# Linear attention and two feed-forward blocks on one core: weight loads, output copies and a normalisation placed earlier in their queues

## The reference

```python
# attention with decay, per head: blocks of 64 tokens, a state carried from block to block
intra = einsum(einsum(qb, kb) * Dmask, vb);  inter = einsum(qb * lam_pow, kv_state)
out[block] = intra + inter
kv_state = lam_block * kv_state + einsum(kb * rev_pow, vb)
# first feed-forward block, on x of shape (2, 768, 512)
mixed = real(fft(fft(x, axis=1), axis=2))
u = x + mixed
un = (u - mean(u)) / sqrt(var(u) + 1e-6)
x1 = u + maximum(un @ w_ch1, 0) @ w_ch2          # 512 -> 2048 -> 512
# second feed-forward block
xn = (x1 - mean(x1)) / sqrt(var(x1) + 1e-6) * g_ln
y = x1 + maximum(xn @ w_ch1', 0) @ w_ch2'
```

## Time and profile before

| | |
|---|---|
| three runs, us | 577.79, 576.11, 578.07 |
| median | 577.79 |
| profiled execution, its own time | 577.79 |
| span of the profiled execution | 575.6 |
| PE busy | 565.5 us (98%) |
| PE weight loads | 390.2 us (68%) |
| DVE busy | 355.9 us (62%) |
| ACT busy | 245.6 us (43%) |
| POOL busy | 167.2 us (29%) |
| DMA engines | nearly full to 86 us; 59.85 MB moved in all |

### The profile page before, as it was taken

The page is one execution under the profiler, slowest core; times in us unless marked ns, Lnnn a source line. Parts: engine busy times, 40 slices in busy tenths (PEclk is TensorE's granted clock), DMA queues, the critical chain, the costliest instruction groups (busy, mean ns, idle before and its releaser), DMA issues.

```text
span 575.6 us, 10716 instructions
## 1 busy us (share of the span) xinstructions
PE 565.5 (98%) x4028; PEld 390.2 (68%) x4028; DVE 355.9 (62%) x618; ACT 245.6 (43%) x483; POOL 167.2 (29%) x147
## 2 busy tenths in 40 slices
PE   9899999999999999999999999999999999999997
PEld 5799987665666666666666666666666666666663
DVE  3446898998866776647969676975265533422223
ACT  1245676647763233424456454544232443232231
POOL 0668940775600011012295312620004300000000
PEclk9999999999999999999999999999999999999999
DMA  7999991000247437630235422132000223200001
GB/s 220 395 368 371 398 289 41 2 19 0 38 74 193 120 124 151 147 109 3 74 91 136 121 75 75 36 74 56 1 2 2 54 47 102 74 2 0 1 1 73
DMA packets 78515, 59.85 MB, mean 104 GB/s; under 512 B 39418, under 2 KB 65666, under 8 KB 77060
## 3 DMA queue, kind: packets, MB, share of 16 engines
q1 hardware_dynamic: 76260, 54.49, 33.2%
q10 hardware_dynamic: 1728, 3.15, 1.4%
q0 software_dynamic: 480, 1.57, 0.8%
HBM read 43.73 MB, written 6.30 MB: 87 GB/s over the span
## 4 chain that ended last, share of the span: by engine, by line
PE 79%; DVE 10%; issue 4%; DMA 3%; POOL 2%; ACT 1%; SPq 1%; DVEq 0%; ACTq 0%; POOLq 0%
PE bank L681 36%; PE bank L661 32%; PE bank L478 3%; PE bank L489 2%; PE bank L540 2%; DMA arena<-attn 2%; DVE arena L1341 2%; DVE arena L1179 2%; DVE arena L1181 2%; PE bank L448 2%; DVE arena L1188 1%; PE bank L461 1%; PE bank L605 1%; DVE arena L1306 1%; DVE arena L1386 1%
## 5 line engine op out<-in xcount | busy, mean ns | idle before, releaser
L681 PE MATMUL bank<-arena 128*128 128x512 f16 x1152 | 287.2, 379 | 1.4 <-DVE arena L1188 1.2
L661 PE MATMUL bank<-arena 128*128 128x256 f16 x2016 | 259.2, 273 | 1.0 <-DVE arena L1318 0.4
L661 PEld LDWEIGHTS bank<-arena 128*128 128x128 f16 x2016 | 196.4, 98 | 76.3 <-DVE arena L1386 1.8
L681 PEld LDWEIGHTS bank<-arena 128*128 128x128 f16 x1152 | 112.3, 98 | 88.2 <-DVE arena L1188 1.8
L1341 DVE SCALAR_TENSOR_TENSOR arena<-arena 128x512 f16<-128x512 f32 x96 | 74.1, 772 | 58.9 <-ACT arena L939 58.8
L939 ACT ACTIVATE arena<-arena 128x512 f16<-128x512 f32 x96 | 60.4, 629 | 104.7 <-DVE arena L1386 99.3
L1380 DVE SCALAR_TENSOR_TENSOR arena<-bank,arena 128x256 f32<-128x256 f32 x48 | 20.2, 421 | 62.3 <-PE bank L661 62.1
L1570 POOL TENSOR_TENSOR arena<-arena 128x512 f32<-128x512 f32 x12 | 18.6, 1570 | 88.8 <-DVE arena L1306 88.8
L1318 DVE TENSOR_TENSOR arena<-arena 128x512 f16<-128x512 f32 x42 | 34.3, 827 | 10.2 <-ACT arena L916 9.9
L991 ACT ACTIVATE arena<-bank 128x256 f32<-128x256 f32 x48 | 18.2, 380 | 48.6 <-PE bank L661 48.6
L1386 DVE SCALAR_TENSOR_TENSOR arena<-bank,arena 128x256 f32<-128x256 f32 x48 | 20.2, 420 | 25.9 <-PE bank L661 25.9
(11 more groups left out here) (112 smaller groups left out, 536.3 us busy)
## 6 DMA issues: line engine op xcount, KB each, us to landing
arena<-w SPq DMA_DIRECT2D x48, 256.0 KB, 4.2
arena<-w SPq DMA_DIRECT2D x24, 512.0 KB, 4.9
arena<-attn SPq DMA_DIRECT2D x10, 1024.0 KB, 8.4
out<-arena SPq DMA_DIRECT2D x12, 256.0 KB, 2.4
arena<-attn SPq DMA_DIRECT2D x4, 512.0 KB, 4.3
x_near<-arena ACTq DMA_DIRECT2D x6, 256.0 KB, 6.2
x_far<-arena ACTq DMA_DIRECT2D x6, 256.0 KB, 6.1
arena<-c SPq DMA_DIRECT2D x1, 1153.5 KB, 9.1
```

The lines of the kernel that those rows point to most:

```text
L661: last = nc.tensor.matmul(bank_, wst[:, i, wx, w, kt, :], xs[s % 2][:, x, ux, :, kt, :], start=not started and k == 0, stop=k == 5, skip_g ...
L681: last = nc.tensor.matmul(ops[t][:], hT[n % 2][:, half, hx, t * P:(t + 1) * P], wdn[:, i, wx, half * DM:(half + 1) * DM], start=first and ...
```

## The change

Four edits. (1) SP: each block c from 2 on gets two chunks of w1, chunk 2(c - 2) behind its queries and keys, chunk 2(c - 2) + 1 behind its values, so every chunk is issued one place earlier. (2) ACT: in units 0 to 5 `x_rows` stands ahead of `expand`. The table of magnitudes is replaced by one chunk per unit from unit 3, with chunks 6 and 7 at unit 9. (3) ACT, pair 4: the four `normal` tiles stand behind the copies of p1 and p7, instead of behind the two splits of the hidden rows. (4) ACT and DVE: block 0 of the next group is split in pair 4 behind the copy of p6, instead of in pair 5 behind that of p7.

```diff
-X_FIRST = {4: (1,), 5: (3,), 6: (5,)}, {5: (0, 1), 6: (3,), 7: (5,)}
-X_SECOND = {3: (0,), 4: (2,), 5: (4,), 6: (6,)}, {5: (2,), 6: (4,), 7: (6,)}
+X_FIRST = {4: (1,), 5: (3,), 6: (5,)}, {5: (1,), 6: (3,), 7: (5,)}
+X_SECOND = {3: (0,), 4: (2,), 5: (4,), 6: (6,)}, {4: (0,), 5: (2,), 6: (4,), 7: (6,)}
-MAGNITUDES = {3: (0,), 5: (1,), 6: (2,), 7: (3,), 8: (4, 5), 9: (6, 7)}
...
                 load_qk(c)
-                if c > 2:
-                    load_up(sp, 0, 2 * c - 5, wraw[0][:, 2 * c - 5, :], w_chunk_in[0][2 * c - 5])
+                load_up(sp, 0, 2 * (c - 2), wraw[0][:, 2 * (c - 2), :], w_chunk_in[0][2 * (c - 2)])
...
                 load_kv(c)
-                load_up(sp, 0, 2 * c - 4, wraw[0][:, 2 * c - 4, :], w_chunk_in[0][2 * c - 4])
+                load_up(sp, 0, 2 * (c - 2) + 1, wraw[0][:, 2 * (c - 2) + 1, :], w_chunk_in[0][2 * (c - 2) + 1])
                 if c == NBLK - 1:
-                    load_up(sp, 0, SLOTS - 1, wraw[0][:, SLOTS - 1, :], w_chunk_in[0][SLOTS - 1])
...
             for u in range(UNITS - 1):
-                if u < UNITS - B:
+                if u < B * HALF:
+                    x_rows(u)
                     expand(u)
-                x_rows(u)
-                for c in MAGNITUDES.get(u, ()):
-                    magnitude(0, c)
+                else:
+                    if u < UNITS - B:
+                        expand(u)
+                    x_rows(u)
+                if 3 <= u < 3 + SLOTS - 1:
+                    magnitude(0, u - 3)
+                if u == 2 + SLOTS - 1:
+                    magnitude(0, SLOTS - 1)
...
                 if n in LATE:
                     q_rows(LATE[n])
+                if n == 4:
+                    normal((0, 1))
                 act.wait_ge(p7_done, n + 1)
...
                     q_rows(4)
+                if n == 4:
+                    normal((2, 3))
...
                 hidden_hi(n, 1)
-                if n == 4:
-                    normal((0, 1))
...
                 hidden_hi(n, 0)
-                if n == 4:
-                    normal((2, 3))
```

## The result

| | before | after |
|---|---|---|
| median of 8 runs each, us | 577.84 | 581.63 |
| lowest to highest | 576.11 to 579.25 | 579.75 to 582.33 |
| ratio after / before | | 1.006 [1.0046, 1.0074] |
| profiled execution, its own time | 577.79 | 582.56 |
| its span | 575.6 | 580.8 |

The changed kernel is slower by 0.6%: +3.8 us by the medians, +3.5 by the ratio, whose interval reaches from 2.7 to 4.3. The forecast was +2.7 (580.5), slower. The time lies in the range. The terms behind it are another matter, and most of what follows is about them. The profiled execution, at 582.56, is slower than each of the eight.

The account below looks back on a forecast made before the run. TensorE (PE) sets the end, busy 98% of the span, so only its waits count. Terms 0.7 + 0.1 + 2.4 - 0.5 = +2.7 on 577.79 gave 580.5 us, range 577.6 to 582.9.

Parts of the forecast that it names:

- Term C: Normalised tiles in pair 4: ACT waits for shift, holding p7's eviction, so PE's p4 and p5 start late; +2.4 us.
- Term D: Feed-forward: POOL works in pair 4; PE waits 0.85 us in pair 5, not 1.33 in pair 6; -0.5 us.
- first rival: Pair 4's hold costs 2.4, pair 6's wait goes without successor, loads arrive in time: +1.1 us, 578.9, no change; chance 0.20.
- Term A: Attention: earlier w1 loads and x writes delay query/key and key/value blocks, so PE waits; +0.7 us, from 0 to 1.6.
- the deadlines: Attention: slack between landing and PE's first read of query/key blocks; landing 1.4 us later makes PE wait 0.55 for block 5.
- third rival: Attention loads not served in issue order, key/value block 1 delayed: +2.0 us, 581.8; chance 0.10 together with the high ends.
- Term B: First feed-forward group: POOL's last folds end later and meet DVE's first weight split; +0.1 us, from 0 to 0.5.
- second rival: Pair 4: DVE reaches shift 2.4 us earlier, all four waits of the first group go: -2.2 us, 575.6; chance 0.08.

Follow-up runs that it names:

- early shift: Pair 4's tile and block 0 moves, plus DVE's row_scale ahead of pair 3's w1 split, against the kernel before: 580.12 us against 579.91, ratio 1.0000.
- feed-forward run: Only pair 4's tile and block 0 moves, attention as before, against the kernel before: 580.33 us against 578.21, ratio 1.0019.

## Why the prediction was right, and where it was not

**What bounds the kernel.** Right: each change of PE's waits in the first group reached the end unchanged (3.0 us at pair 7, 3.0 at the last pair). The span grew by 5.2; the other 2.2 lie behind DVE's last instruction, where the last writes land (2.5 and 4.7 us). That part takes either of two lengths from one execution to the next, as said above, so one trace of each kernel can't put it down to the change.

**Term C (+2.4).** Right, mechanism and size. Tiles at shift's end, idle time put down to DVE, the p4 group 6.39 us after its pair's start where about 6.4 was forecast. The wait was 1.99 ahead of p4 and 0.20 ahead of p5; the pair grew by 2.56 with the clock at 1.0, in three traces (12.61 to 12.63). The early shift shows the cause. What the term lacked is the clock: in the first trace it fell to 0.50 after the wait and cost 1.3 more. No row of the trace of before could have given that, as the clock holds in its pairs.

**Term D (-0.5).** Sign right, size wrong: -1.40, just past the low end of its range, and the wait in pair 5 that it foresaw did not come. The step that failed is "POOL works at 141.7 to 148 instead, beside DVE's splits in pair 4". Only t1 moved. The chunk 7 sums behind it wait for DVE's split of chunk 5, which in pair 4 comes after the hold. In the second trace of the changed kernel, with the clock steady, PE wanted the w2 split at 149.70, where the forecast puts it (148.55, and 1.12 for the later start of pair 4), but the split ended at 149.20, and not at 150.5 (149.4, and 1.12). From the product eviction on, DVE took 5.2 us, not 6.6. In the kernel before, that split was done at 142.9 and POOL reached the sums only at 147.7, so its trace shows no wait there. But one chunk earlier it does, and the order could have been read from it (L1550 is the first sum of a chunk, L1181 the second half of DVE's w1 split):

```profile
134.07 1.05 POOL L1550 TENSOR_TENSOR arena<-arena 128x256 f32<-128x256 f32 x1 [0.94 <-DVE arena L1181]
```

The forecast took POOL's work as one block and left out what each of its instructions waits for. The first rival, which said that the wait of pair 6 goes without a successor, had this part right (and had given POOL's unchanged amount of work as the reason against it).

**DVE against POOL.** By the rule of the Trainium skill, "SBUF — State Buffer", section "Who interferes with whom", that a DVE instruction with two SBUF inputs and a GpSimd instruction that reads SBUF exclude each other, the prediction estimated about 2 us of wait in pair 5. No run shows one, as POOL did not work beside DVE's w1 split there. On the rule itself the prediction misread its row ("The row speaks for some overlap"). The lengths overlap, but the ends follow each other. POOL's sum of the earlier trace rows ends at 154.33 + 1.72 = 156.05, and DVE's split of the earlier trace rows at 157.13, 1.08 later: nearly the whole 1.28 that it takes alone still lay ahead of it. In the changed kernel POOL's L1553 ends at 148.23, DVE's L1191 at 149.31 (1.08 later), and POOL's L1554 at 149.89 (0.58 later; such a sum takes 0.72 alone). So the time for which an instruction is held lies inside its length.

All 14 traces say the same. In the first feed-forward group, a DVE instruction with both operands in SBUF (a split) began beside a running POOL instruction 138 times. In 112 of them it ended a fixed time after POOL did: 1.07 to 1.10 us for 1024 columns, 0.80 to 0.82 for 768, 0.53 to 0.56 for 512. In the other 26 DVE was done first, and POOL, though begun earlier, ended 0.58 to 0.60 after it. Here the two engines took turns, and the traces agree with the Trainium skill. DVE's evictions, which take one operand from PSUM, were not held: 104 of them that began beside POOL took 0.40 to 0.43, as L1383 at 142.66 beside L1586. The 6.9 us that the sum took from pair 5 of the kernel before held this taking of turns already, so the estimate of 2 us of wait counted part of it twice.

**Term A (+0.7).** Not seen, and not excluded. (The working itself comes to 0.6, since it says that the two delays don't add; 0.7 is a slip.) Edit 1 alone gives 0.9996, the rows' edit alone 0.9997, each with an interval of about 1 us to either side, and the Fourier part starts at the same mean time in traces with and without edit 1. The scores of block 5 stood at 52.86, and the prediction had named 52.8 as a sign of being wrong. The failing step is the deadlines: slacks of 1.5, 1.5 and 0.85 us were read from one execution. PE was to wait for block 5 and nowhere else; in the changed kernel it waited 0.31, 0.53 and 0.38 for blocks 3, 4 and 5. In others, with the order of loads of before, PE waits for blocks 4 and 5 too (0.46 and 0.67 in the feed-forward run). Landings vary by more than what the edit moves. Nor does the write of x, priced at 0.6 us ahead of key/value block 1, show: in the changed kernel PE's row group started at 20.83, 1.4 earlier than before, and over all traces its mean start is the same with and without the edit. For the third rival (+2.0 for the loads and writes) there is no sign either; edit 1's interval ends at +0.9.

**Term B (+0.1).** Pair 2 starts 49.8 us after the Fourier part in before and 50.3 in the changed kernel. Over all traces it is 50.4 with edit 1 (50.27 to 50.90) and 50.1 without (49.79 to 50.37), so about +0.3, within its bounds, but no more than single traces differ.

**The sum.** By the traces with a steady clock: A 0, B +0.3, C +2.56, D -1.40, together +1.5 where +2.7 was forecast. Measured were +3.5 (2.7 to 4.3) and +2.3 (1.4 to 3.1): +1.5 lies at the low end of the second and under the first. So the forecast came out close by luck. It had 0.7 too much for A and 0.9 too much for D, and no term for the clock. The mean granted clock over all executions was 0.9974 for the changed kernel (0.9989 for the kernel before on the first chip of the experiments), and 0.9959 against 0.9984 on the second chip. 0.0025 x 580 = 1.5 us is an estimate of the most that this can cost on the second chip, and it would close the gap there (+2.3 against 1.5). For the first result 0.0015 x 580 = 0.9 us would not. Nor can the clock be all of it: of the 25 executions of the changed kernel on record, eight have a mean clock of 0.999 or more, and they average 580.5, still 2.7 above the 577.84 of the kernel before (the clocks of those runs are not on record). What the rest is stays open; the longer end behind DVE's last instruction is a candidate, as no kernel with the hold was traced without it. That the hold costs clock in other executions is argued, not shown: only one was traced with the fall in pair 4. The kernels with the hold (changed, feed-forward part, tiles alone) have mean clocks of 0.996 to 0.997, most of the others 0.998 to 0.999, but the kernel with the rows' edit alone has 0.9965 with no hold and no loss of time, and one with the tiles behind the w1 split 0.997. Whether the hold makes falls more frequent stays open.

**Faster (second rival).** Its condition, shift earlier against PE, was set up in the run with the early shift. The hold went, as it says, but making shift early cost 0.75 in pair 3, and no gain was measured. A gain was had the other way, with the tiles behind the w1 split, where shift is always there already: 1.0 us.

## What to carry to other kernels

An instruction that waits for another engine, placed in a queue ahead of a short copy that the bounding engine needs, holds that engine too: here ACT stood for 3.29 us, and PE's pair grew by 2.56. The same work placed behind all that others need soon gained 1.0 us. When work is moved earlier, read the waits of everything behind it on each engine it releases, since the next semaphore may keep it where it was. And a slack of a microsecond against a DMA landing, read in one execution, is not a number to build a term on: compare it in several traces first. Where two engines exclude each other, don't read overlapping lengths as overlapping work: compare their ends.

## What the runs showed of the hardware

TensorE's granted clock fell from 1.0 to 0.50 right after a 2.0 us wait in one execution (142 to 144 us, 1.3 us lost), and stayed at 1.0 after the same wait in three others (the changed kernel again, and the two kernels with the tiles between the copies). Those three had each had a fall in attention already, between 18 and 22 us, where PE had waited about 0.9 us for a load; the first had had none. Whether an earlier fall matters for a later one, these four traces can't say. Nor does the length of the wait in attention decide alone: PE waits for a load ahead of its scores at 17 to 19 us in all 14 traces. Six have the fall, after waits of 0.88 to 1.25 us, and eight have none, after waits of 0.53 to 0.96 (0.96 in the kernel before).

The same loads, issued in the same order, let PE into the Fourier part at 63.4 us in one execution and at 66.4 in another. That spread of 3 us is as large as the effect of the whole change. It need not be landings alone: the later one had the fall of the clock in attention, the earlier one had not. The six traces with the fall enter at 65.6 on average, the eight without at 64.6; how much of that 1.0 is the clock and how much the landings isn't told apart.

DVE instructions with both operands in SBUF and POOL instructions took turns in the first feed-forward group, and each shows its blocked time as part of its length: 1.28 us alone, 1.75 and 2.29 beside POOL. DVE's evictions with an operand in PSUM kept their 0.40 to 0.43 us.

The time from DVE's last instruction to the end of the span was 2.5 us in four traces and 4.0 to 4.7 in ten, and kernels with edits stand in both groups.
